# Loading alpha, k and q without their unused rows in an attention, token-mixing and gated-FFN kernel

## What is computed

```python
B, H, S, D = q.shape                      # 4, 8, 768, 48
state = np.zeros((B, H, D, D))
for t in range(S):
    state = alpha[:, :, t, :, None] * state + np.einsum('bhd,bhe->bhde', k[:, :, t], v[:, :, t])
    y[:, :, t] = np.einsum('bhd,bhde->bhe', q[:, :, t], state)
```

## Time and profile before

| | us |
|---|---|
| runs of the kernel before | 532.6, 534.77, 534.57 |
| median | 534.57 |
| the profiled execution, device time | 532.05 |
| its span, first to last instruction | 530.3 |
| VectorE busy in the span | 441.2 |
| TensorE busy in the span | 521.7 |

### The profile page before, as it was taken

How to read it: one execution, slowest core, us unless ns; L and a number is a source line. 1 busy time by engine, 2 the same in 40 slices (tenths; PEclk the granted TensorE clock), 3 DMA queues, 4 the chain that set the end, 5 groups by cost and what they waited for, 6 DMA issues and landing times.

```text
span 530.3 us, 11805 instructions
## 1 busy us (share of the span) xinstructions
PE 521.7 (98%) x4142; PEld 512.8 (97%) x4142; DVE 441.2 (83%) x801; ACT 287.4 (54%) x607; POOL 72.0 (14%) x65
## 2 busy tenths in 40 slices
PE   7999999999999999999999999999999999999997
PEld 7999888999999999999999999999999999999997
DVE  8999997998886759767786787999888888889874
ACT  4888888765534434444244553555555454545353
POOL 5988983000000000000000000000000000000000
PEclk9999999999999999999999999999999999999999
DMA  8899997476131020211062011202020110201011
GB/s 326 303 328 327 314 340 228 140 229 214 38 104 31 17 70 28 92 30 54 15 210 89 1 45 58 77 2 90 0 89 32 57 55 34 89 0 47 0 46 45
DMA packets 37163, 56.93 MB, mean 107 GB/s; under 512 B 3328, under 2 KB 27392, under 8 KB 37120
## 3 DMA queue, kind: packets, MB, share of 16 engines
q1 hardware_dynamic: 34000, 51.65, 29.3%
q10 hardware_dynamic: 3120, 4.72, 2.5%
HBM read 42.20 MB, written 14.16 MB: 106 GB/s over the span
## 4 chain that ended last, share of the span: by engine, by line
PE 91%; SPq 2%; DMA 2%; issue 2%; ACT 1%; DVE 1%; POOL 0%; ACTq 0%; DVEq 0%
PE y_bank L1474 26%; PE y_bank L1533 19%; PE theta_bank L1520 10%; PE x_bank L1520 10%; PE y_bank L1504 7%; PE theta_bank L1461 7%; PE weighed L1371 4%; PE x_sum L1328 3%; PE x_sum L1343 2%; PE turned L1357 2%; PE x_bank L1449 1%; SPq L731 1%; DMA x_in<-x_scratch 1%; PE turned L1376 1%; PE x_sum L1314 1%
## 5 line engine op out<-in xcount | busy, mean ns | idle before, releaser
L1533 PE MATMUL y_bank<-first_w,z 128*128 128x384 f32 x576 | 109.5, 335 | 0.0
L1533 PEld LDWEIGHTS y_bank<-first_w,z 128*128 128x128 f32 x576 | 101.2, 188 | 0.0
L1474 PE MATMUL y_bank<-first_w,z 128*128 128x384 f32 x432 | 78.0, 337 | 0.1
L1474 PE MATMUL y_bank<-rest_w,z 128*128 128x384 f32 x432 | 76.9, 336 | 0.0
L1474 PEld LDWEIGHTS y_bank<-first_w,z 128*128 128x128 f32 x432 | 74.5, 188 | 0.3 <-issue 0.3
L1474 PEld LDWEIGHTS y_bank<-rest_w,z 128*128 128x128 f32 x432 | 74.7, 188 | 0.0
L1042 ACT ACTIVATE out_rows<-theta_bank 128x386 f32<-128x386 f32 x32 | 15.8, 493 | 50.6 <-PE theta_bank L1520 50.5
L1273 DVE TENSOR_SCALAR x_rows<-out_rows,taps 128x384 f32<-128x384 f32 x64 | 26.8, 419 | 19.5 <-ACT out_rows L1042 19.4
L1461 PE MATMUL theta_bank<-theta_w,x_t 128*128 128x384 f32 x216 | 41.6, 336 | 0.1
L1276 DVE SCALAR_TENSOR_TENSOR x_rows<-out_rows,taps,x_rows 128x384 f32<-128x384 f32 x64 | 39.6, 619 | 2.3
L1280 DVE SCALAR_TENSOR_TENSOR z_full<-out_rows,taps,x_rows 128x384 f32<-128x384 f32 x64 | 39.6, 619 | 2.3
(11 more groups left out here) (126 smaller groups left out, 974.2 us busy)
## 6 DMA issues: line engine op xcount, KB each, us to landing
a_in<-in_a_rows SPq DMA_DIRECT2D x15, 390.0 KB, 5.7
k_in<-in_k_rows SPq DMA_DIRECT2D x15, 384.0 KB, 5.3
q_in<-in_q_rows SPq DMA_DIRECT2D x14, 384.0 KB, 5.2
v_in<-in_v_tokens SPq DMA_DIRECT2D x16, 288.0 KB, 4.7
x_in<-x_scratch SPq DMA_DIRECT2D x24, 192.0 KB, 2.6
y<-x_all SPq DMA_DIRECT2D x7, 576.0 KB, 3.3
u_scratch<-u_sum ACTq DMA_DIRECT2D x6, 576.0 KB, 3.5
u_first<-u_scratch SPq DMA_DIRECT2D x4, 577.5 KB, 4.4
```

Of the source, the lines that this page charges most:

```text
L1474: ins = pe.matmul(y_bank[2 * d + half][:, 0:HALF], z[s % 2][part][zp][:, d * P:(d + 1) * P], mixing_w(part, wp, s)[:, half_tokens(half)], ...
L1533: ins = pe.matmul(out_bank[half][t][:, 0:MODEL], g[k % 4][gp][:, t * P:(t + 1) * P], out_w[wp][f], start=f == 0 and i == 0, stop=f == FF_T ...
```

## The change

The 48 dimensions of a head no longer fill the first 48 partitions of its slot but three of every four: dimension d goes to partition 4*(d//3) + d%3, and every fourth partition (3, 7, ..., 127) is filler. The first load into each buffer still brings all 128 rows, so that the filler is set once. Every later load of alpha, k or q is two transfers, one of the 64 even rows and one of the 32 rows 1, 5, 9, ..., 125; rows 3, 7, ... keep what they had. Both transfers add 16 to the same semaphore, which so counts by 32, and SyncE adds the missing 16 once to each of the eight semaphores at the start. The loads concerned are those of alpha from pair 4 on, and of k and q from pair 2 on: 12 + 14 + 14 = 40 loads become 80 transfers.

```diff
+ROWS_OF_HEAD = [4 * (d // 3) + d % 3 for d in range(HEAD_DIM)]
...
-    got_a = [count(f"got_a{u}", 16) for u in range(4)]
-    got_k, got_q = ([count(f"got_{x}{u}", 16) for u in range(2)] for x in "kq")
+    got_a = [count(f"got_a{u}", 32) for u in range(4)]
+    got_k, got_q = ([count(f"got_{x}{u}", 32) for u in range(2)] for x in "kq")
...
         def rows(tiles, source, got, n):
-            sp.dma_start(tiles[n % len(tiles)][:, :], source[n, :, :]).then_inc(got[n % len(tiles)].sem, 16)
+            u = n % len(tiles)
+            if n < len(tiles):
+                sp.dma_start(tiles[u][:, :], source[n, :, :]).then_inc(got[u].sem, 16)
+            else:
+                for used in (slice(0, P, 2), slice(1, P, 4)):
+                    sp.dma_start(tiles[u][used, :], source[n, used, :]).then_inc(got[u].sem, 16)
...
         rows(a_in, a_rows, got_a, 2)
+        for got in (got_a, got_k, got_q):
+            for t in got:
+                sp.sem_inc(t.sem, 16)
...
-    out[:, :, 0:HEAD_DIM] = rows.reshape(PAIRS, 2, HEAD_DIM, -1)
+    out[:, :, ROWS_OF_HEAD] = rows.reshape(PAIRS, 2, HEAD_DIM, -1)
```

More of the change, by code:

```diff
@@ L127, in source @@
             if x == "a":
-                return a_rows.rearrange("n (g d) (c s) -> n g d c s", g=2, s=SPAN)[n, g, 0:HEAD_DIM, :, 1:CHUNK + 1]
+                return a_rows.rearrange("n (g d) (c s) -> n g d c s", g=2, s=SPAN)[n, g, :, :, 1:CHUNK + 1]
             if x == "v":
                 return v_rows.rearrange("(n g) d (c t) -> n g d c t", g=2, t=CHUNK)[n, g, :, :, :]
-            return {"k": k_rows, "q": q_rows}[x].rearrange("n (g d) (c t) -> n g d c t", g=2, t=CHUNK)[n, g, 0:HEAD_DIM, :, :]
+            return {"k": k_rows, "q": q_rows}[x].rearrange("n (g d) (c t) -> n g d c t", g=2, t=CHUNK)[n, g, :, :, :]
         def path(sp):
@@ L141, in path @@
                     for g in range(2):
-                        sp.dma_start(self.rows[x][g * SLOT:g * SLOT + HEAD_DIM, :].rearrange("p (c t) -> p c t", t=CHUNK),
+                        used = HEAD_DIM if x == "v" else SLOT
+                        sp.dma_start(self.rows[x][g * SLOT:g * SLOT + used, :].rearrange("p (c t) -> p c t", t=CHUNK),
                                      source(x, n, g)).then_inc(self.got.sem, 16)
@@ L841, in first_pair @@
         def first_pair():
-            for chunks, k_got, q_got, a_done, k, b_done, q in (
-                    (AHEAD, first_k_got, first_q_got, first_after, first_k, first_before, first_q),
-                    (BEHIND, got_k[0].sem, got_q[0].sem, after_done.sem, k_done.sem, before_done.sem, q_done.sem)):
+            for chunks, a_done, k, b_done, q in (
+                    (AHEAD, first_after, first_k, first_before, first_q),
+                    (BEHIND, after_done.sem, k_done.sem, before_done.sem, q_done.sem)):
                 pool.wait_ge(a_done, 1)
-                pool.wait_ge(k_got, 16)
+                if chunks is AHEAD:
+                    pool.wait_ge(first_k_got, 16)
+                else:
+                    got_k[0].done(pool, 0)
                 pool.tensor_tensor(chunked(k_scaled[0][:, :])[:, chunks, :], chunked(k_in[0][:, :])[:, chunks, :],
@@ L850, in first_pair @@
                 pool.wait_ge(b_done, 1)
-                pool.wait_ge(q_got, 16)
+                if chunks is AHEAD:
+                    pool.wait_ge(first_q_got, 16)
+                else:
+                    got_q[0].done(pool, 0)
                 pool.tensor_tensor(chunked(q_scaled[0][:, :])[:, chunks, :], chunked(q_in[0][:, :])[:, chunks, :],
```

## The result

| | before | changed |
|---|---|---|
| runs, us | 532.6, 534.77, 534.57, 531.05 | 541.08, 543.75, 540.33, 541.99 |
| median, us | 533.59 | 541.54 |
| ratio, 95% interval | | 1.0168 (1.0146 to 1.019) |
| span of the profiled execution, us | 530.3 | 539.4 |
| VectorE busy in the span, us | 441.2 | 441.4 |

The change makes the kernel 1.7% slower, 8 to 9 us. I had forecast 534.0 with a range up to 538.5.

What follows compares the result with a forecast made beforehand. VectorE, at 4.83 us per pair-loop step, was taken as the bound. Bytes gave -0.5 us, other terms 0: 532.05 - 0.5 = 531.55 for the profiled execution, forecast as 534.0 on the median; own range 532.3 to 535.8, full range 531.5 to 538.5.

Steps and rivals of the forecast that it cites:

- VectorE sets the period, traffic does not stretch it.: In the loop over head pairs, VectorE runs without gaps, 4.83 us a step, whatever the DMA traffic.
- Bytes are worth 0.5 us.: Fewer bytes gain nothing mid-loop; shorter DMA waits at the loop's end gain 0.5 us, out of 0 to 1.2.
- Loads would land in 3 to 4 us.: Loads of alpha, k and q land 3 to 4 us after issue instead of 5.2 to 5.7.
- Three more transfers cost SyncE 1.44 us in a turn.: Three added transfers per loop step at 0.48 us each; SyncE's turn with normal issues becomes 4.16 us, within 4.84.
- Long issues of 0.67 us in a turn.: Overlong SyncE issues between 34 and 66 us, 4.7 us in seven turns, bring the average turn to 4.83 us.
- 0 us, since slack of landing absorbs the rest.: k's second transfer must land within 4.9 us, 3 to 4 expected for the pair; 0 us, range 0 to 1.5 loss.
- the two signs named for this: SyncE's x_made waits near nothing with scans further apart would show the queue rival; GpSimd's 1.26 us k wait should go.
- queue rival: SyncE's turn exceeds 4.83 us, long issues growing from 0.67 to 1.0 us; about 537.3 us, chance 0.13.
- The rival of strided rows: Transfers to every second or fourth partition run at half rate, 0.7 us over VectorE's period; about 542 us, chance 0.11.
- The Trainium skill's rule.: Use one 128-partition transfer, not two to disjoint halves; by it the sum would be a loss, by the rows a small gain.

## Why the prediction was wrong

- *VectorE sets the period, traffic does not stretch it.* Right: the scans take 1768 to 1780 ns in the changed kernel, and up to 49 us they follow each other every 4.83 us. After that SyncE's turn sets the pace.
- *Bytes are worth 0.5 us.* Right in that it is next to nothing: half of the bytes gave 0.9 to 1.4 us, a quarter without more transfers no gain. The 0.5 itself is not shown.
- *Loads would land in 3 to 4 us.* Right, 3.1 to 3.4.
- *Three more transfers cost SyncE 1.44 us in a turn.* This is the step that failed. It took 0.48 us from the kernel's transfers of 128 and 48 rows, and the new ones have 64 and 32. They measured: k 1.11 instead of 0.43, q 1.12 instead of 0.42, alpha 1.18 instead of 0.40, and the neighbours v 0.58 instead of 0.33 and two stores 1.05 instead of 0.90. The sum is 2.56 us, so the clean turn is 2.72 + 2.56 = 5.28 instead of 4.16 (5.33 measured). With 4.16 there was slack for the long issues; with 5.3 the queue is over VectorE's period even without them, in every turn.
- *Long issues of 0.67 us in a turn.* They stayed, at about 5.80 - 5.33 = 0.47. They did not grow with the number of instructions, as the rival had it, nor vanish with the traffic.
- *0 us, since slack of landing absorbs the rest.* The landing slack is a stock that is used up once. The v load of 47.19 came 3.8 us later than its like of 43.41 before, and VectorE had lost nothing yet; that is why the steps up to 49 us look so harmless. The v load of 76.91 came 8.7 us later than that of 68.20, and VectorE had lost 7.1 us by its mask at 77.80: from 49 us on the loss grew with the backlog, not evenly but in the turns with long issues. Of the two signs named for this, the first came: waits for x_made near nothing and scans further apart, which stood for the queue rival. The other, GpSimd's wait for k gone, did not: before its k scaling at 51.89 stand 1.33 us, where it had been 1.26 at 50.44. (The window of that k load is 49.18 - 43.84 = 5.34 us, not 5.4; nothing hangs on it.)
- *The rivals.* The queue rival had the right place and the right sign (deciding from a turn over 4.83 us) but was priced at 537.3 since it rested on the same 0.48. With 5.80 - 4.83 = 0.97 in ten turns it comes to 9.7 us, before its own allowance for loads that land earlier. I also gave it 0.13, though my own sum had put the queue at exactly 4.83 us, without slack: an edit that adds work to a resource at its limit deserves more. The rival of strided rows would have given a time (542) nearer to the result, for the wrong reason: in the changed kernel the loads land sooner, and spread rows are the faster ones.
- *The Trainium skill's rule.* "Don't bother" in "DMA: Bandwidth & Descriptors", section "Rules for kernel authors", came out right for this change, and the sum by it (a loss) was the better one. But the reason that it gives, that both transfers use the same DMA engines, is not what made the loss here: the loads landed sooner, and the 2.56 us of issuing on SyncE did it.

## What to carry to other kernels

Before a transfer is split, add up the issuing queue's own turn: number of transfers times the time that each takes to issue, against the period of the engine that sets the pace. A queue that waits 1.7 us in a turn looks idle and is full after three more transfers; and a price for an issue holds for the shape that it was read from. Saving bytes gained next to nothing where the engine that sets the pace never waited for a load; its first effect is a shorter landing, which is worth only what somebody waited.

## What the runs showed of the hardware

- The time that a queue needs for a transfer depends on its number of rows, and not in the way of bytes: 0.40 to 0.45 us for 48, 96 or 128 rows, about 0.6 for 64 (adjacent or every second) and for 32 rows (every fourth, the only form tried), all rows of some 3 KB or, in stores, 1.5 KB. A part of it appears at the next transfer: a store takes 0.58 us behind 32 rows and 0.42 behind another store. Why 48 rows are cheaper than 64 stays open.
- A set of adjacent partitions can be slower to fill than a spread one: halves of 64 adjacent rows landed alpha in 6.3 us, even and odd rows in 3.9. With single transfers of 64 rows and half of the bytes the difference is smaller, 4.4 against 3.8 us. And rows 0 to 95 in one transfer landed no sooner (5.8) than 0 to 127 (5.6). The Trainium skill, "SBUF — State Buffer", section "Door 1: The DMA port swizzle", agrees: by it, the first 64 partitions lie behind half of the 16 ports, so leaving out rows 96 to 127 takes nothing from the busiest ports, while leaving out every fourth row takes a quarter from each.
- The long issues on SyncE (up to 2.62 us for two stores before, 2.40 for two alpha transfers after) appear in each kernel in its loaded stretch. What they are was not tried.
